# A fused attention, expert and mixing kernel: the high part of a head's keys in three pieces, and five smaller edits of order and division of work

## What is computed

```python
# 1: banded attention, B=2, H=8 heads, S=768, D=64
scores = q @ k.T / 8 - slope[h] * dist;  keep = (k_pos < 8) | (0 <= rel < 96)
x = (softmax(where(keep, scores, -1e9)) @ v)          # rows of B*S = 1536 tokens, 512 wide
# 2: one expert of eight per token; a token may keep the expert of the one before it
e = argmax(x @ w_gate) if (s == 0 or sigmoid(x @ w_local) < 0.5) else prev_e
y = softmax(x @ w_gate)[e] * (relu(x @ w1[e]) @ w2[e])
# 3: mixing
theta = y @ w_theta
u = y + w_tok_r @ (y * cos(theta)) + w_tok_i @ (y * sin(theta))
out = u + relu(u @ w_ch)
```

## Time and profile before

| | |
|---|---|
| median of 3 runs | 513.42 us (512.89 to 514.06) |
| the profiled execution | 513.58 us, of which the span is 510.7 us |
| mean granted clock of TensorE in the span | 0.987 |
| PE busy, PEld busy | 492.2 us (96%), 430.5 us (84%) |
| DVE, ACT, POOL busy | 275.1 us, 205.5 us, 101.9 us |
| first scores; end of the last turn-back | 11.3 us; 99.1 us |
| routing, to the first expert matmul | 99.1 to 119.4 us |
| expert tiles; mixing | 119.4 to 328 us; 328 to 510.7 us |

### The profile page before, as it was taken

How to read it: one execution, slowest core, us unless ns; L and a number is a source line. 1 busy time by engine, 2 the same in 40 slices (tenths; PEclk the granted TensorE clock), 3 DMA queues, 4 the chain that set the end, 5 groups by cost and what they waited for, 6 DMA issues and landing times.

```text
span 510.7 us, 9337 instructions
## 1 busy us (share of the span) xinstructions
PE 492.2 (96%) x3356; PEld 430.5 (84%) x3356; DVE 275.1 (54%) x642; ACT 205.5 (40%) x422; POOL 101.9 (20%) x113
## 2 busy tenths in 40 slices
PE   9899999759999999999999999999999999999997
PEld 8788888549999999999999999877888878888885
DVE  5688888774115141424423421778877675444243
ACT  4978887312114141414414454645553242222010
POOL 3998680011111111111111111000000000000000
PEclk9999999958999999999999999999999999999999
DMA  8645318623949283838947301050000000000012
GB/s 334 237 150 198 124 53 332 239 64 114 390 165 349 103 331 116 313 129 309 377 192 285 115 24 41 24 207 0 2 1 0 1 0 22 21 22 21 22 62 82
DMA packets 20696, 71.14 MB, mean 139 GB/s; under 512 B 2734, under 2 KB 5806, under 8 KB 16432
## 3 DMA queue, kind: packets, MB, share of 16 engines
q1 hardware_dynamic: 17872, 63.88, 33.2%
q0 software_dynamic: 2640, 6.30, 3.5%
q10 hardware_dynamic: 144, 0.44, 0.2%
HBM read 62.49 MB, written 10.49 MB: 143 GB/s over the span
## 4 chain that ended last, share of the span: by engine, by line
PE 84%; DVE 10%; issue 4%; ACT 2%; DVEq 0%; ACTq 0%
PE ps L1385 44%; PE ps L1414 22%; PE ps L1240 4%; PE ps L1317 3%; PE ps L1280 3%; PE ps L1300 2%; PE ps L1255 2%; PE ps L1401 1%; PE ps L1489 1%; PE ps L1450 1%; DVE raw L959 1%; ACT z_hi L810 1%; DVE z L1158 1%; DVE x_tok L1190 1%; DVE z_lo L1135 1%
## 5 line engine op out<-in xcount | busy, mean ns | idle before, releaser
L1414 PEld LDWEIGHTS ps<-xT,w_sb 128*128 128x128 f32 x1024 | 116.7, 192 | 1.8 <-DVE xT L1130 0.6
L1414 PE MATMUL ps<-xT,w_sb 128*128 128x128 f32 x1024 | 117.0, 275 | 0.4 <-DVE xT L1130 0.4
L1116 DVE SCALAR_TENSOR_TENSOR hT_lo<-ps,hT_hi 128x512 fp32r<-128x512 f32 x32 | 22.1, 690 | 98.1 <-ACT hT_hi L743 98.0
L1125 DVE TENSOR_TENSOR w_lo<-w_sb,w_hi 128x1024 fp32r<-128x1024 f32 x32 | 37.0, 1220 | 38.9 <-ACT w_hi L773 38.9
L688 ACT ACTIVATE prob<-raw,row_min 128x256 f32<-128x256 f32 (+1 forms) x96 | 45.9, 480 | 14.5 <-DVE row_min L959 14.5
L1385 PE MATMUL ps<-w_hi,hT_hi 128*128 128x512 f32 x128 | 51.2, 400 | 0.0
L1385 PE MATMUL ps<-w_lo,hT_hi 128*128 128x512 f32 x128 | 49.9, 390 | 0.0
L1385 PE MATMUL ps<-w_hi,hT_lo 128*128 128x512 f32 x128 | 49.9, 390 | 0.0
L743 ACT ACTIVATE hT_hi<-ps 128x512 fp32r<-128x512 f32 x32 | 19.1, 597 | 72.5 <-PE ps L1414 72.5
L749 ACT COPY yout<-ps 128x512 f32<-128x512 f32 x16 | 9.4, 587 | 71.1 <-PE ps L1385 71.1
L773 ACT CAST w_hi<-w_sb 128x1024 fp32r<-128x1024 f32 x32 | 31.1, 1044 | 12.5 <-DVE first_tile L1101 12.5
(11 more groups left out here) (178 smaller groups left out, 945.1 us busy)
## 6 DMA issues: line engine op xcount, KB each, us to landing
w_sb<-in_w_experts SPq DMA_DIRECT2D x32, 1024.0 KB, 7.9
v_sb<-in_vx SPq DMA_DIRECT2D x8, 640.0 KB, 4.1
q_raw<-in_q SPq DMA_DIRECT2D x8, 384.0 KB, 5.4
x_tok<-y_rows SPq DMA_DIRECT2D x12, 256.0 KB, 4.5
out_x<-o_sb SPq DMA_DIRECT2D x12, 256.0 KB, 2.0
k_raw<-in_kx SPq DMA_DIRECT2D x7, 432.0 KB, 4.7
x_rows<-x_tok SPq DMA_DIRECT2D x2, 1152.0 KB, 11.1
wtr<-in_w_tok_rT SPq DMA_DIRECT2D x6, 384.0 KB
```

The costliest lines, as they stand in the source:

```text
L1116: dve.scalar_tensor_tensor(hT_lo[:, part, :], ps[:, 1 + half, :].rearrange("p (c q) -> p c q", c=4), 0.0, hT_hi[:, part, :].bitcast(F32), ...
L1125: dve.tensor_tensor(quarter(w_lo, par, q), quarter(w_sb, par, q), w2_hi_quarter(q).bitcast(F32), ALU.subtract).then_inc(s_w2_lo, 1)
L1414: last = pe.matmul(ps[:, 1 + half, f * P:(f + 1) * P], w_sb[:, par, c // 2, j:j + P], xT[:, c, :], start=(c == 0), stop=(c == DC - 1))
```

## The change

What it does, edit by edit:

1. ACT makes the high keys of a head in three pieces and not two, and no longer all at once: `key_pieces` gives the 32 first keys of all windows (128x192), the rest of windows 0 to 2 (128x672), the rest of windows 3 to 5 (128x672). For head h they come at the end of rounds 3h-5, 3h-4 and 3h-3. POOL makes the low part piece by piece, with a wait before each piece. Heads 0 and 1 are made in three pieces too, but together.
2. At rounds 4, 7, ..., 22 PE issues the turn-back between the values of tile 0 and those of tile 1.
3. Turn-back 13 goes to PSUM bank 0, waits for `s_raw` of all tiles but the last in place of `s_x_done`, and comes before the values of its round.
4. At the start DVE makes the low keys and low queries of head 0 before the distances; 26 blank matmuls in place of 36.
5. In the routing ACT makes 3 of the 12 `at_place` tiles, each with two activations and a wait between them (Abs, then Relu); the token numbers are counted from the end.

```diff
+BY_SCALAR = 3
+PIECES = 3
+def key_pieces(keys, raw):
+    start = window_parts(keys, raw, 0, QT)[1]
+    return [start, window_parts(keys, raw, 0, GROUP)[0], window_parts(keys, raw, GROUP, QT)[0]]
+def ready_values(r):
+    if r == PAIRS // 2 - 1:
+        return 0
+    return 1 if r >= 4 and (r - 1) % 3 == 0 else QT
 def back_bank(q):
-    return 3 if q == LAST else 7
+    return {LAST: 3, LAST - 2: 0}.get(q, 7)
 ...
         def keys_low(eng, h):
-            for (low, whole), (high, _) in zip(window_parts(k_lo[:, r, :], k_raw[:, r, :], 0, QT),
-                                               window_parts(k_hi[:, r, :], k_raw[:, r, :], 0, QT)):
+            for j, ((low, whole), (high, _)) in enumerate(zip(key_pieces(k_lo[:, r, :], k_raw[:, r, :]),
+                                                              key_pieces(k_hi[:, r, :], k_raw[:, r, :]))):
+                eng.wait_ge(s_k_hi, PIECES * h + j + 1)
                 last = eng.tensor_tensor(low, whole, high.bitcast(F32), ALU.subtract)
 ...
-                pool.wait_ge(s_k_hi, h + 1)
                 keys_low(pool, h)
 ...
-            def keys_high(h):
+            def keys_high(h, first, last):
-                for where, whole in window_parts(k_hi[:, r, :], k_raw[:, r, :], 0, QT):
-                    last = act.copy(where, whole)
-                last.then_inc(s_k_hi, 1)
+                for where, whole in key_pieces(k_hi[:, r, :], k_raw[:, r, :])[first:last]:
+                    act.copy(where, whole).then_inc(s_k_hi, 1)
 ...
-                    if r % 3 == 1 and r // 3 + 2 < H:
-                        keys_high(r // 3 + 2)
+                    h, piece = (r - 1) // 3 + 2, (r - 1) % 3
+                    if r and h < H:
+                        keys_high(h, piece, piece + 1)
 ...
+            act.wait_ge(s_in_tile, 1)
+            for j in range(BY_SCALAR):
+                n = NT - BY_SCALAR + j
+                act.activation(distance[:, j, :], con("place"), ACT.Abs, bias=home[:, 0, n:n + 1],
+                               scale=-1.0).then_inc(s_distance, 1)
+                act.wait_ge(s_distance, j + 1)
+                act.activation(at_place[:, n, :], distance[:, j, :], ACT.Relu, bias=con("from_end")[:, n:n + 1],
+                               scale=con("token")[:, n:n + 1]).then_inc(s_at_place_act, 1)
 ...
-            distances(con("rel_near"), con("key_near"), NARROW.start, levels[:, 0], (0, 1), s_ch, s_mask)
-            dve.wait_ge(s_k_hi, 1)
+            distances(con("rel_near"), con("key_near"), NARROW.start, s_ch)
             keys_low(dve, 0)
             dve.wait_ge(s_q_hi, 1)
             dve.tensor_tensor(q_lo[:, 0, :], q_raw[:, 0, :], q_hi[:, 0, :].bitcast(F32),
                               ALU.subtract).then_inc(s_q_split, 1)
+            by_distance(con("key_near"), levels[:, 0], (0, 1), s_mask)
 ...
-            for n in range(NT):
+            for n in range(NT - BY_SCALAR):
 ...
-            keep_running(36, 5)
+            keep_running(26, 5)
 ...
-                if q == LAST:
+                if bank == 0:
+                    pe.wait_ge(s_raw, B * (PAIRS - 1))
+                elif bank == 3:
                     pe.wait_ge(s_raw, B * PAIRS)
                 else:
                     wait(pe, s_x_done, q)
 ...
-                    for g in values_at(r):
+                    ready = ready_values(r)
+                    for g in values_at(r)[:ready]:
                         values(g)
                     for q in turned_back_at(r):
-                        turn_back(q)
+                        turn_back(q, back_bank(q))
+                    for g in values_at(r)[ready:]:
+                        values(g)
```

More of the change, by code:

```diff
@@ L63 @@
 _WIDTHS = [("numbers", 2), ("key_near", WINDOW), ("rel_near", NARROW.stop - NARROW.start), ("ident", P), ("before", P), ("ones", P), ("first", NT), ("erev", NT * E), ("starts", E * NT),
-           ("carry", E * NT), ("place", P), ("token", NT), ("tile", NT * MAP)]
+           ("carry", E * NT), ("place", P), ("token", NT), ("from_end", NT), ("tile", NT * MAP)]
 COL, _at = {}, 0
@@ L92, in constants @@
     put("token", p + np.arange(NT)[None] * P - NO_TOKEN)
+    put("from_end", NO_TOKEN - p - np.arange(NT)[None] * P)
     put("tile", np.tile(np.arange(MAP), NT)[None])
@@ L244, in program @@
         s_at_place = sem("at_place")
+        s_distance = sem("distance")
+        s_at_place_act = sem("at_place_act")
         s_g_act = sem("g_act")
@@ L382, in program @@
         at_place = sb("at_place", [P, NT, P], F32R)
+        distance = sb("distance", [P, BY_SCALAR, P])
         in_tile = sb("in_tile", [P, NT, MAP], F32R)
@@ L669, in keys_high @@
                 wait(act, s_scores, QT * (h - 1))
[L670 to L674 removed]
+                for where, whole in key_pieces(k_hi[:, r, :], k_raw[:, r, :])[first:last]:
+                    act.copy(where, whole).then_inc(s_k_hi, 1)
+            keys_high(0, 0, PIECES)
             act.wait_ge(q_in[0], 16)
@@ L705, in exponentials @@
                         exponential(g, b, width(g))
-                keys_high(1)
+                keys_high(1, 0, PIECES)
                 exponentials(0)
@@ L723, in whole_rows @@
                     if g % QT == 0 and g:
-                        keys_high(g // QT)
+                        keys_high(g // QT, 0, PIECES)
                     for b in range(B):
@@ L859, in _, with distances @@
             then(dve.tensor_scalar(scaled[:], nloc_f[:, 1:2], FIRST_SLOPE, None, ALU.mult))
-            def distances(rel, key, at_rel, to, tiles, chain, done):
+            def distances(rel, key, at_rel, chain):
                 keys, rels = key.shape[1], rel.shape[1]
@@ L870, in distances, with by_distance @@
                 then(dve.tensor_tensor(near[:, c], tmp_m[:, c], rel, ALU.subtract), chain)
+            def by_distance(key, to, tiles, done):
+                g, keys = glob[:, 0:key.shape[1]], key.shape[1]
                 for at_, i in enumerate(tiles):
@@ L926, in normalise @@
                 h, half = q // 2, q % 2
-                if q < LAST - 1:
+                if q < LAST - 2:
                     dve.wait_ge(s_back, q + 1)
-                shares(q, half, h % 2, tiny if q < LAST - 1 else tiny_s[:])
+                shares(q, half, h % 2, tiny if q < LAST - 2 else tiny_s[:])
                 logits(q, half, back_bank(q))
@@ L980, in whole_rows @@
                 dve.wait_ge(s_rest_in, 16)
-                distances(far[:, 0:REL], far[:, REL:], 0, dist, range(QT), s_ch_all, s_mask_all)
+                distances(far[:, 0:REL], far[:, REL:], 0, s_ch_all)
+                by_distance(far[:, REL:], dist, range(QT), s_mask_all)
                 def rows_of_head(h, last):
@@ L1093, in _ @@
                               ALU.is_equal).then_inc(s_in_tile, 1)
-            for n in range(NT):
-                dve.tensor_scalar(at_place[:, n, :], con("place"), place[:, n:n + 1], con("token")[:, n:n + 1],
+            for n in range(NT - BY_SCALAR):
+                dve.tensor_scalar(at_place[:, n, :], con("place"), place[:, n:n + 1], con("from_end")[:, n:n + 1],
                                   ALU.is_equal, ALU.mult).then_inc(s_at_place, 1)
@@ L1102, in _ @@
             dve.wait_ge(s_inverse, 1)
-            dve.tensor_scalar(token_at[:, 1:], ps[:, 3, 0:MAP], float(NO_TOKEN), None, ALU.add).then_inc(s_map, 1)
+            dve.tensor_scalar(token_at[:, 1:], ps[:, 3, 0:MAP], -1.0, float(NO_TOKEN), ALU.mult, ALU.add).then_inc(s_map, 1)
             then(dve.tensor_reduce(total_p, gate_f[:], AX.X, ALU.add))
@@ L1266, in room_for_values, with turn_back @@
                         wait(pe, s_ot1, q // 2)
-            def turn_back(q):
+            def turn_back(q, bank):
                 if q % 2:
@@ L1279, in turn_back @@
                 for j in range(GROUP):
-                    last = pe.matmul(ps[:, back_bank(q), j * TURNED:(j + 1) * TURNED], outT[:, q % 2, j * P:(j + 1) * P],
+                    last = pe.matmul(ps[:, bank, j * TURNED:(j + 1) * TURNED], outT[:, q % 2, j * P:(j + 1) * P],
                                      wg[:, q // 2, :], start=True, stop=True)
@@ L1361, in whole_rows @@
                     if i % GROUP == GROUP - 1:
-                        turn_back(g // GROUP)
+                        turn_back(g // GROUP, back_bank(LAST) if g == PAIRS - 1 else 7)
             either(pe, which_path(pe), windows, whole_rows)
@@ L1391, in _ @@
             for n in range(NT):
-                pe.wait_ge(s_at_place, n + 1)
+                if n < NT - BY_SCALAR:
+                    pe.wait_ge(s_at_place, n + 1)
+                else:
+                    pe.wait_ge(s_at_place_act, n - NT + BY_SCALAR + 1)
                 last = pe.matmul(ps[:, 3, 0:MAP], at_place[:, n, :], in_tile[:, n, :], start=(n == 0), stop=(n == NT - 1))
```

1 line of the change is left out of this document (removed).

## The result

The changed kernel takes 514.67 us (median of 7 runs, 514.52 to 515.96), the kernel before 513.01 us beside it (7 runs, 512.37 to 514.06). The ratio is 1.0037, 95% interval 1.0022 to 1.0051: slower by 1.7 us, where 1.2 us faster was forecast. The profiled execution has a span of 512.8 us against 510.7.

A forecast was written before the change was run, and what follows sets the result against it. PE, busy 96% of the span, was taken as nearly full. 513.58 + 0.1 (start and attention) - 0.95 (last turn-backs) - 0.35 (routing) gave 512.4 us profiled, 512.2 median; range 508.6 to 513.9.

The forecast's parts named there:

- the ring: Attention heads: low keys, q_hi, lg, raws, ACT's pieces and POOL's low part follow in a loop of 10.93 us a head.
- Rival 1: Attention: q_hi does not hold lg, or POOL is elsewhere; a head takes 10.21, the kernel 508.8 us; chance 0.18.
- The 1.3 us won at head 2: Head 2's first scores come at 28.0 instead of 29.3, with one piece in ACT's way at round 1.
- The start: Second head's scores at 18.65, first raw at 19.25: no gain for what follows.
- E: The end of a head's low keys on POOL; for the second head put at 18.55 (18.3 to 18.9).
- an unheld head: Attention head whose lg does not wait for q_hi: without PE's 0.39 us stop at tile 1's values it takes 10.21 us.
- 1.4 won: Attention: gain in us from taking away four stops of PE at the values of tile 1.
- +0.1: Start and attention up to head 7's scores: 1.3 and 1.4 us won, all given back; range -0.7 to +0.8.
- -0.95: End of attention: turn-back 13 follows the transposes at once, so all behind moves 0.95 us earlier (0.7 to 1.0).
- -0.35: Routing: DVE makes 9 tiles instead of 12, so the end comes 0.35 us earlier (-0.8 to +0.3).
- I take 0.13 each, since only 20 columns move: Routing: the last three matmuls, in a row behind DVE's ninth tile at half clock, cost 0.13 us each.
- Scores of the second head later than 18.9: Sign in the changed profile, at the start of attention, that would show the start was mis-sized.

The follow-up runs named there:

- e2_lg_psum: The changed kernel with one of lg's two SBUF inputs moved to PSUM for the first 12 turn-backs, and lg put ahead of the rows of x: 513.70 us.
- e3_pieces_alone: The kernel before with only the high keys made in three pieces spread over three rounds: 513.94 us.
- e4_start_undone: The changed kernel with the new start order undone (distances first, 36 blank matmuls): 513.46 us.
- e7_edit2_alone: The kernel before with only the turn-back put between the values of tiles 0 and 1 in rounds 4, 7, ..., 22: 512.84 us.
- e12_edits3_5: The kernel before with only turn-back 13 in bank 0 and three routing tiles on ACT: 512.18 us.
- e8_edits3_5_weights: The kernel before with turn-back 13 in bank 0, two routing tiles on ACT, and the first expert's weights loaded earlier: 511.74 us.
- e13_quiet: The changed kernel with head 2's loads held until DVE's first raw, and the gate weights and far constants moved behind them: 512.65 us.

## Why the prediction was wrong

- **Edit 1, the ring: right.** `q_hi` holds lg (0.83, not 1.3: see edit 2), a turn takes 10.89 (predicted 10.93), five turns 54.46 (predicted 82.4 - 28.0 = 54.4). The rule of the Trainium skill (SBUF — State Buffer, Who interferes with whom) that I had weighed against the row for q_lo holds for q_hi too, and e2_lg_psum shows it from the other side. Rival 1 fell. The 1.3 us won at head 2 are 1.5 in e3_pieces_alone.
- **The start, edit 4: this step failed.** I wrote that the scores of head 1 come at 18.65, right behind E, and asked only what delays E. E was right (18.46). I had priced what edit 4 moves on DVE, but not what its earlier splits release on SP, the loads of head 2, nor who else uses the DMA queues then. Measured: h1 +1.60 against the forecast, h2 +2.12. Of the further 0.5, 0.3 is edit 2's split at round 4, and 0.3 a wait of the values at 24.03 for ACT's outT, which e4_start_undone has too (0.31) without DVE's stop; its cause stays open. From there the difference stays: +2.18 at head 7.
- **Edit 2: mis-sized, in the model of an unheld head.** The 0.39 of the earlier trace rows is a real stop, but taking it away costs PE 0.30 for the added change between kinds of matmul, a term that the prediction put at nothing. "Without it the head would take 10.21" is 10.53 (e7_edit2_alone). In the ring it hides, since the turn there goes over ACT and POOL; of the "1.4 won" four heads give 0.3, and rounds without a stop take that back. So the prediction's split of the +0.1 was wrong, and that its sum was not is luck.
- **Edit 3: right.** -0.95 forecast, -1.0 in e12_edits3_5. The changed kernel shows -0.8, because the split of edit 2 at round 22 costs 0.2 there.
- **Edit 5: mis-sized.** -0.35 forecast, -0.1 measured. The step that failed is "I take 0.13 each, since only 20 columns move": at half clock the three matmuls behind the ninth are 0.22 apart, hardly less than DVE's 0.256 a tile, so three tiles win 0.12 and the two of e8_edits3_5_weights 0.08. ACT's operations take 0.40 and 0.49, not 0.36, but ACT is not waited for, 0.29 late behind DVE as it is.
- **Missing from the sum:** +0.9 behind attention, since the branch there meets full queues. The late start is not what it takes: e13_quiet starts in time, issues the weights at 78.46 (78.14 before, 80.48 in the changed kernel) and has the same 1.62 between gate_m and PE. In both, the last turn-back ends 20.16 us behind the issue of the weights, where it was 21.02: attention's end moved towards the transfers. How much of this is edit 3 is not shown; e12_edits3_5 has 20.01 and loses only 0.2, e3_pieces_alone 20.65 and loses 0.4. I had read the earlier trace rows and the gather, but never the idle time of ACT at 97 to 100 us marked "issue".

In sum: 509.5 us of span by the forecast, +2.2 at head 7, +0.15 for round 22, +0.9, +0.25 for edit 5 make 513.0; measured 512.8, with a gather that happened to be 0.5 shorter and 0.3 more behind it. "Scores of the second head later than 18.9 would show that the start was mis-sized" is what came. The range ended at 513.9, since no case had a stop that isn't a wait.

## What to carry to other kernels

Where an edit releases transfers earlier, ask not only who waits for the data but what else must come over the same queues: an engine at or behind a branch needs code, and here stood, with no releaser in the profile, until the data ahead of it were through. Idle time marked "issue" beside or just behind a DMA share near 1.00 was the sign; moving a load that nobody needs yet was the cure, worth 0.8 us at one branch and up to 2 at the other. And before a stop of 0.4 is taken away by reordering a full engine's work, price the added change of kind by rows with and without it, in every round where it is made: here it was 0.30, against a stop of 0.38 in four of seven rounds.

## What was not expected of the hardware

- Code behind data: stops of 2.48 (DVE, some instructions behind a branch), 3.50 (PE) and 5.35 us (ACT) beside a DMA share of 0.82 to 1.00; none, a wait for DVE, and 2.02 us once the queues were quiet. In e13_quiet DVE's first raw behind a branch stood for 1.14 us at a DMA share of 0.00; that the branch is the reason was not tested.
- A DVE tensor_tensor with both inputs in SBUF is held to the end of POOL's instruction beside it: 0.83 to 1.12 beside `q_hi`, 2.21 beside a large `k_lo`; 0.21 beside `q_hi` with one input in PSUM, 0.20 with POOL at rest.
- Splitting twelve matmuls of values by a turn-back costs PE 0.30 us with no wait in sight (2.92 against 2.62 us for the same 26 matmul records).
- On ACT a 128x128 activation takes 0.40 (Abs) to 0.49 us (Relu with scale and bias from a tile), as much as one of 128x256 with its row sums.
